# Clustered attention and two mixers: packed one-hot transposes, weighted sums a step later, similarities in one step, denominators per head

## The reference

```python
q_assign = argmax(q_n @ c_n.T)          # per head: 16 clusters, 768 queries, 64 dimensions
k_assign = argmax(k_n @ c_n.T)
mask = q_assign[:, None] == k_assign[None, :]
scores = where(mask, q @ k.T / sqrt(64), -1e9)
attn = softmax(scores)                  # per row
out = attn @ v
```

## Time and profile before

| what | value |
|---|---|
| median of 3 runs | 699.2 us (699.09 to 701.43) |
| the profiled execution | 700.45 us, span of its records 698.6 us |
| TensorE's mean granted clock | 0.993 of full speed |
| busy, share of the span | TensorE 97%, VectorE 56%, ScalarE 48%, GpSimd 27% |
| the attention stage | from some 16 us to 281.5 us |

### The profile page before, as it was taken

How to read it: one execution, slowest core, us unless ns; L and a number is a source line. 1 busy time by engine, 2 the same in 40 slices (tenths; PEclk the granted TensorE clock), 3 DMA queues, 4 the chain that set the end, 5 groups by cost and what they waited for, 6 DMA issues and landing times.

```text
span 698.6 us, 11568 instructions
## 1 busy us (share of the span) xinstructions
PE 679.3 (97%) x4188; PEld 643.6 (92%) x4188; DVE 391.5 (56%) x673; ACT 338.5 (48%) x641; POOL 191.8 (27%) x140
## 2 busy tenths in 40 slices
PE   7999999999999998999999999999999999999998
PEld 6888898989898987889999999999999999999998
DVE  6698888888897988445212202403268626671133
ACT  4687878787978788424401201301277425530010
POOL 5558253443535374402600000200223200060000
PEclk8999999999999999999999999999999999999999
DMA  6474644535353451100300000010231100000022
GB/s 218 87 177 122 170 100 103 135 68 135 68 135 68 100 149 46 32 14 20 125 9 0 1 1 0 0 45 1 59 122 50 57 1 1 0 1 1 1 90 91
DMA packets 16016, 45.44 MB, mean 65 GB/s; under 512 B 2544, under 2 KB 4592, under 8 KB 15984
## 3 DMA queue, kind: packets, MB, share of 16 engines
q1 hardware_dynamic: 15984, 45.00, 23.9%
HBM read 24.15 MB, written 3.15 MB: 39 GB/s over the span
## 4 chain that ended last, share of the span: by engine, by line
PE 87%; ACT 4%; DVE 4%; issue 3%; DMA 0%; ACTq 0%; DVEq 0%; SPq 0%
PE ps L439 19%; PE ps L441 19%; PE ps L440 19%; PE ps L477 7%; PE ps L485 5%; PE ps L469 4%; PE ps L486 4%; PE ps L470 4%; PE ps L450 3%; PE ps L461 1%; DVE pt_lo L1067 1%; ACT pt_hi L758 1%; ACT prob L783 1%; ACT kb L778 1%; PE ps L492 1%
## 5 line engine op out<-in xcount | busy, mean ns | idle before, releaser
L1039 DVE TENSOR_REDUCE neg_max<-ps 128x1 f32<-128x768 f32 x96 | 91.5, 954 | 27.4 <-PE ps L470 24.5
L1067 DVE TENSOR_TENSOR pt_lo<-ps,pt_hi 128x384 fp32r<-128x384 f32 x192 | 97.5, 549 | 11.2 <-ACT pt_hi L758 10.8
L758 ACT ACTIVATE pt_hi<-ps 128x384 fp32r<-128x384 f32 x192 | 84.4, 489 | 38.1 <-PE ps L477 36.6
L783 ACT ACTIVATE prob<-ps,neg_max 128x768 f32<-128x768 f32 x96 | 86.7, 904 | 13.1 <-DVE neg_max L1039 11.9
L867 ACT ACTIVATE g_s<-ps 128x384 fp32r<-128x384 f32 x48 | 23.6, 492 | 139.4 <-PE ps L441 139.4
L441 PE MATMUL ps<-u_s,ch_s 128*128 128x384 f32 (+1 forms) x256 | 85.5, 334 | 0.0
L439 PE MATMUL ps<-u_s,ch_s 128*128 128x384 f32 (+1 forms) x256 | 85.5, 334 | 0.0
L440 PE MATMUL ps<-u_s,ch_s 128*128 128x384 f32 (+1 forms) x256 | 85.5, 334 | 0.0
L477 PE MATMUL ps<-ident,prob 128*128 128x128 f32 x576 | 82.9, 278 | 1.4 <-DVE pt_lo L1067 1.3
L477 PEld LDWEIGHTS ps<-ident,prob 128*128 128x128 f32 x576 | 67.0, 143 | 10.6 <-DVE pt_lo L1067 2.7
L485 PE MATMUL ps<-pt_lo,v_s 128*128 128x384 f32 x192 | 70.2, 366 | 4.8 <-DVE o_sum L1046 4.8
(11 more groups left out here) (143 smaller groups left out, 1419.7 us busy)
## 6 DMA issues: line engine op xcount, KB each, us to landing
stage<-ch_dram SPq DMA_DIRECT2D x9, 768.0 KB, 4.3
qa<-pair_s SPq DMA_DIRECT2D x30, 192.0 KB, 2.8
ka<-pair_s SPq DMA_DIRECT2D x30, 192.0 KB, 3.8
raw<-q_dram SPq DMA_DIRECT2D x8, 384.0 KB, 4.2
raw<-k_dram SPq DMA_DIRECT2D x8, 384.0 KB, 4.6
raw_v<-v_dram SPq DMA_DIRECT2D x8, 384.0 KB, 4.3
out_dram<-act_u SPq DMA_DIRECT2D x16, 192.0 KB, 1.9
qb<-pair_s SPq DMA_DIRECT2D x15, 192.0 KB, 3.4
```

What stands on the lines that cost most here:

```text
L758: return act.activation(o, i, ACT.Copy)
L783: act.activation(prob[:, slot, :].rearrange("p (c k) -> p c k", c=2), ps[:, 2 * slot:2 * slot + 2, 0:HS], ACT.Exp, bias=neg_max[:, s:s + 1 ...
L1039: dve.tensor_reduce(neg_max[:, s:s + 1], ps[:, 2 * slot2:2 * slot2 + 2, 0:HS], AX.XY, ALU.max, negate=True).then_inc(s_max, 1)
L1067: dve.tensor_tensor(pt_lo[at], ps[:, 4 + u, 0:HS].rearrange("p (k q) -> p k q", k=HT), pt_hi[at], ALU.subtract).then_inc(s_pt_lo, 1)
```

## The change

- `onehot` has 32 columns for each of the four combinations of head and side, 16 of them always zero, so that one transpose of 128 columns gives the rows of both heads and both sides. One group of six per pair is left, behind the transposes of step 7.
- ScalarE copies all 128 rows at once to a new tile `oh_rows` (`rows_out`, with scale and bias from small per-partition tiles, function Identity), and SyncE's `oh_in` copies 16 rows each to qb and kb of the two heads: four transfers a pair. Only for the very first head the rows are still copied by ScalarE itself.
- In TensorE's order part 0 of `weighted_v` goes from the end of steps t = 0 and 3 to steps t = 1 and 4, between the scores and the transposes; part 1 goes from the end of t = 1 and 4 to the start of t = 2 and 5, ahead of the scores.
- Both sides of `sims` are in step 3, one ahead of the transposes and one behind. VectorE's argmax steps go from steps 3, 4, 5, 6, 7 to 3, 3, 3, 4, 6.
- rden holds the six tiles of a head, made at t = 0 of the next head by `denominators`; `x_out` waits for that and for s_x_bank.

```diff
-                onehot = sb(a1, "onehot", [P, 2, NT, 2, C], BF16)
+                onehot = sb(a1, "onehot", [P, NT, 2, 2, 2 * C], BF16)
+                oh_rows = sb(a1, "oh_rows", [P, S], F32R)
...
+            def oh_in(p, j):
+                sp.wait_ge(s_oh_rows, p + 1)
+                for dst, side in ((qb, 0), (kb, 1)):
+                    r = j * D + side * 2 * C
+                    sp.dma_start(dst[D:D + C, j, :].bitcast(F32), oh_rows[r:r + C, :].bitcast(F32)
+                                 ).then_inc(s_oh_in[j], 16)
+
...
+                oh_in(p + 1, 0)
                 sp.wait_ge(s_score, 12 * p + 12)
                 stack(p + 1, 1)
+                oh_in(p + 1, 1)
 
...
-                pool.wait_ge(s_rden, n + 1)
+                pool.wait_ge(s_x_bank, n + 1)
+                pool.wait_ge(s_rden, 2 * p + j + 1)
                 pool.tensor_tensor(x_tok[:, bass.ds(p * NT + half * HT, HT), j * D:(j + 1) * D], o_sum[:, half, :, :],
-                                   rden[:, half, :].unsqueeze(2).broadcast_to([P, HT, D]),
+                                   rden[:, j, half * HT:half * HT + HT].unsqueeze(2).broadcast_to([P, HT, D]),
                                    ALU.mult).then_inc(s_x, 1)
 
...
+                    pe.wait_ge(s_oh_rows, p)
                     pe.wait_ge(s_cen_t, 4)
                     pe.wait_ge(s_qk_c, p)
...
-            def oh_transpose(j, side, bank=7):
-
-                rows = ps[D:D + C, bank, 0:HS].bitcast(BF16)
+            def oh_transpose(bank=7):
+
+                rows = ps[:, bank, 0:HS].bitcast(BF16)
                 for t in range(NT):
-                    mm = pe.transpose(rows[:, t * P:(t + 1) * P], onehot[:, side, t, j, :], identb[:])
+                    mm = pe.transpose(rows[:, t * P:(t + 1) * P],
+                                      onehot[:, t, :, :, :].rearrange("p j s c -> p (j s c)"), identb[:])
                 mm.then_inc(s_oh_t, 1)
 
...
+            def second_half_v(n, j, part):
+
+                pe.wait_ge(s_pt_lo, 6 * n - 1 + part)
+                if part == 0:
+                    pe.wait_ge(s_x_bank, n - 1)
+                weighted_v(1 - j, 1, part)
+
+            def first_half_v(p, n, j, part, prev):
+
+                pe.wait_ge(s_pt_lo, 6 * n + 5 + part)
+                if part == 0:
+                    pe.wait_ge(s_v_split, 2 * p + j + 1)
+                    if prev:
+                        pe.wait_ge(s_x_bank, n)
+                weighted_v(j, 0, part)
 
             def pair(p, first=False, last=False):
                 for s in range(12):
                     j, t = s // NT, s % NT
                     g = 12 * p + s
                     n = 4 * p + 2 * j
+                    prev = not (first and j == 0)
+                    if t == 2 and prev:
+                        second_half_v(n, j, 1)
+                    if t == 5:
+                        first_half_v(p, n, j, 1, prev)
                     if not (last and s >= 10):
                         next_score(p, s + 2)
-                    if s == 0:
-                        pe.wait_ge(s_koh, 2 * p + 1)
-                        oh_transpose(1, 0)
                     if s == 3 and not last:
-                        sims(p + 1, 1)
-                    prev = not (first and j == 0)
+                        sims(p + 1, 0)
+                    if t == 1 and prev:
+                        second_half_v(n, j, 0)
+                    if t == 4:
+                        first_half_v(p, n, j, 0, prev)
                     pe.wait_ge(s_exp, g + 1)
                     for u in range(2):
                         if not (first and s == 0):
                             pe.wait_ge(s_pt_lo, 2 * g + u - 1)
                         transposes(g, s % 2, u)
-                    if s == 1:
-                        pe.wait_ge(s_qoh, 2 * p + 2)
-                        oh_transpose(1, 1)
-                    if s == 2 and not last:
-                        pe.wait_ge(s_koh, 2 * p + 2)
-                        sims(p + 1, 0)
-                    if s == 8 and not last:
+                    if s == 3 and not last:
+                        sims(p + 1, 1)
+                    if s == 7 and not last:
                         pe.wait_ge(s_onehot, p + 3)
-                        oh_transpose(0, 0)
-                    if s == 9 and not last:
-                        pe.wait_ge(s_qoh, 2 * p + 3)
-                        oh_transpose(0, 1)
+                        oh_transpose()
                     if (t == 2 and prev) or t == 5:
                         pe.wait_ge(s_ot, n if t == 2 else n + 1)
                         o_transpose()
-
-                    if prev and t < 2:
-                        pe.wait_ge(s_pt_lo, 6 * n - 1 + t)
-                        if t == 0:
-                            pe.wait_ge(s_x_bank, n - 1)
-                        weighted_v(1 - j, 1, t)
-                    if t in (3, 4):
-                        pe.wait_ge(s_pt_lo, 6 * n + 5 + t - 3)
-                        if t == 3:
-                            pe.wait_ge(s_v_split, 2 * p + j + 1)
-                            if prev:
-                                pe.wait_ge(s_x_bank, n)
-                        weighted_v(j, 0, t - 3)
 
             def idle_work(n):
                 for i in range(n):
...
-            def query_rows(h, j, bank=7):
-                act.wait_ge(s_oh_t, 2 * h + 1)
-                copy(qb[D:D + C, j, :], ps[D:D + C, bank, 0:HS].bitcast(BF16)).then_inc(s_qoh, 1)
-
-            def mask_rows(h, j, bank=7):
-
-                act.wait_ge(s_oh_t, 2 * h + 2)
-                act.activation(kb[D:D + C, j, :], ps[D:D + C, bank, 0:HS].bitcast(BF16), ACT.Copy,
+            def query_rows_first():
+                act.wait_ge(s_oh_t, 1)
+                copy(qb[D:D + C, 0, :], ps[0:C, 6, 0:HS].bitcast(BF16)).then_inc(s_qoh, 1)
+
+            def mask_rows_first():
+
+                act.wait_ge(s_oh_t, 2)
+                act.activation(kb[D:D + C, 0, :], ps[2 * C:3 * C, 5, 0:HS].bitcast(BF16), ACT.Copy,
                                scale=BIG, bias=-BIG).then_inc(s_koh, 1)
+
+            def rows_out(p, bank=7):
+
+                act.wait_ge(s_oh_t, p + 2)
+                act.activation(oh_rows[:], ps[:, bank, 0:HS].bitcast(BF16), ACT.Identity, scale=oh_scale[:, 0:1],
+                               bias=oh_bias[:, 0:1]).then_inc(s_oh_rows, 1)
 
...
-                    if s == 0:
-                        query_rows(2 * p + 1, 1)
-                    if s == 1:
-                        mask_rows(2 * p + 1, 1)
-                    if s == 8 and not last:
-                        query_rows(2 * p + 2, 0)
-                    if s == 9 and not last:
-                        mask_rows(2 * p + 2, 0)
-
-            query_rows(0, 0, bank=6)
-            mask_rows(0, 0, bank=5)
+                    if s == 7 and not last:
+                        if not first:
+                            act.wait_ge(s_oh_in[0], 32 * p)
+                        act.wait_ge(s_oh_in[1], 32 * p + 32)
+                        rows_out(p + 1)
+
+            act.wait_ge(s_oh_zero, 9)
+            query_rows_first()
+            mask_rows_first()
+            rows_out(0, bank=5)
...
+            dve.memset(onehot[:], 0.0).then_inc(s_oh_zero, 1)
+            for r in range(4):
+                rows = slice(2 * C * r, 2 * C * r + 2 * C)
+                dve.memset(oh_scale[rows, :], BIG if r % 2 else 1.0).then_inc(s_oh_zero, 1)
+                dve.memset(oh_bias[rows, :], -BIG if r % 2 else 0.0).then_inc(s_oh_zero, 1)
...
-            def half_out(n, half, j):
+            def half_out(n, half):
 
                 dve.wait_ge(s_ott, n + 1)
-                if half is not None:
-                    dve.tensor_reduce(o_sum[:, half, :, :],
-                                      ps[:, 6, 0:HS].rearrange("p (t a d) -> p t d a", t=HT, a=2), AX.X,
-                                      ALU.add).then_inc(s_x_bank, 1)
-                s = NT * j + HT * half
-                dve.tensor_scalar(rden[:, half, :], den[:, s:s + HT], 1e-9, None, ALU.add).then_inc(s_den, 1)
-                dve.wait_ge(s_den, n + 1)
-                dve.reciprocal(rden[:, half, :], rden[:, half, :]).then_inc(s_rden, 1)
+                dve.tensor_reduce(o_sum[:, half, :, :], ps[:, 6, 0:HS].rearrange("p (t a d) -> p t d a", t=HT, a=2),
+                                  AX.X, ALU.add).then_inc(s_x_bank, 1)
+
+            def denominators(h, j):
+                dve.tensor_scalar(rden[:, j, :], den[:, NT * j:NT * j + NT], 1e-9, None, ALU.add).then_inc(s_den, 1)
+                dve.wait_ge(s_den, h + 1)
+                dve.reciprocal(rden[:, j, :], rden[:, j, :]).then_inc(s_rden, 1)
 
             def pair(p, first=False, last=False):
                 for s in range(12):
                     n = 4 * p + 2 * j
                     if not (last and s >= 10):
                         row_max(g + 2, s % 2, (s + 2) % 12)
-                    if s == 7 and not last:
```

(20 more changed lines are left out.)

45 lines of the change are left out of this document (27 added, 18 removed).

## The result

The changed kernel takes 679.12 us (median of 4 runs, 678.63 to 680.13), the kernel before beside it 699.51 (699.09 to 701.43). The ratio is 0.9711, with a 95% interval of 0.970 to 0.972: 20.4 us less. The prediction said 681.5, 17.7 less than the 699.2 that it started from. The profiled executions, 700.45 and 680.13 us, differ by 20.3.

The account below looks back on a forecast made before the run. TensorE, busy 97% of the span, was taken as the bound. Full pairs save 2.4 x 7 = 16.8 us, the last pair 1.2, the start costs 0.3: 17.7 off 699.2 gives 681.5 us, range 676 to 691.

Parts of the forecast that it names:

- main term: Attention stage: a full pair of heads takes 30.3 us against 32.7, saving 2.4 us in each of seven pairs, 16.8.
- Packed one-hot transposes: TensorE, attention pairs: 32 groups of six transposes become nine, 14.3 us off; wider loads give 0.5 us back.
- ScalarE's copies: ScalarE, row copies: one 1.0 us copy replaces four of 0.80 a pair, 2.2 us less; Identity loads no table.
- Rival 4: ScalarE, row copy: Identity needs another table, two 1.28 us loads a pair; 6 us slower, 705; chance 0.04 including the like.
- Copies by DMA: SyncE's row transfers to qb and kb: landing in 1.9 to 2.5 us, no cost but little room for head 0.
- rival 3: Row transfers come late: landing at 4.1 us costs 1.5 us a pair, 10 us, total 692; chance 0.08.
- wrong if S(12) waits for the rows: Sign against the forecast: the next pair's first score products on TensorE wait for transferred key rows; no such wait was forecast.
- V one step later: TensorE's weighted sums: moving part 0 behind the next scores removes the 0.47 us wait for o_sum at step 6.
- All similarities in step 3: TensorE similarities, VectorE argmax lump: TensorE's 2.5 us a pair stay; waits in a pair 1.0 us, today 1.6.
- Denominators per head: VectorE: two pairs of small instructions instead of four save 0.6 us a pair; GpSimd's later x_out is hidden.
- Start and end: Before the first pair: zeroing onehot (0.5 us) and eight memsets cost 0 to 0.5 us; last pair's end keeps its order.

## Why the prediction was right, and where its working was not

**The total** was 2.4 us from the measured one, and its main term was right in mechanism: the period fell to 29.9, where 30.3 was worked out. In the sum, the group with the stretch of the T ahead stood at 0.7 and takes 0.32, its late start being among the waits; the waits are 0.66 for 1.0. That is 0.7 less. The rest was counted as 26.1 + 2.5 and is 0.3 more: the T between the two sides of the similarities takes 0.68 (120.73 to 121.41) and the S behind them 0.80, and T and O of step 8 take 0.71 and 0.30, where 0.58, 0.71, 0.65 and 0.25 were the prices.

**Step "Packed one-hot transposes"**, 14.3 us off TensorE. The work did go. But that this step pays by itself was wrong with the addition in place: alone it gives 2.3 us, and 12 to 13 without the addition on either side. The working took TensorE's own sum and one estimate of the waits for the whole, and did not ask whether VectorE would still be in time if only TensorE became shorter. The price of the group was bounded by 0.43 and 0.58 and lies below both: the wide load costs less than the narrow one.

**Step "ScalarE's copies".** 1.0 was the estimate, 0.99 the measurement. Identity loads no table. The whole trace has three loads, at 0.74, 16.88 and 490.26 us, as the kernel before has (0.74, 16.12, 511.91). Only the second lies in the attention stage, and the eight Identity copies, one at 15.88 and seven among the exponentials, add none. Rival 4 falls with it.

```profile
16.88 1.28 ACT L811 ACT_TABLE_LOAD   x1
```

The rule of the Trainium skill, page ScalarE: Activation LUTs, section on table sets, was weighed in the prediction; the trace now agrees with it for Identity as well as for copy.

**Step "Copies by DMA"**, "no cost, but little room". Right but for one pair (landing 2.1 us, room 0.3). In the second pair rival 3 happened: landing 5.6 us, a wait of 3.03. By the prediction's own signs ("wrong if S(12) waits for the rows") this pair speaks against it. The working counted the queue from a steady pair; the second pair still has GpSimd's weight splits ahead of split_qk. Its pair takes 33.19, with the weight early 29.87, and so gained 0.5 instead of 2.4.

**Step "V one step later"**, "takes away the 0.47". The place of V is worth 0.47, but that is luck. In the kernel before the move does take away the wait for o_sum; in the changed kernel the order of o_sum and argmax has already done so, and what the move saves is wait of T for pt_lo, which the step said would get no more room. Not foreseen either: the same edit costs 10 us in the kernel before, since V covered the wait for the key rows. In the changed kernel one group at step 7 replaces the two at steps 8 and 9, and the rows are there 0.3 ahead of S(12) without that cover.

**Step "All similarities in step 3"**. T(6), the one-hot group, T(0) and T(9) wait 0.16, 0.26, 0.17 and 0.07, where 0.15, 0.4, 0.2 and 0.2 were counted. The lump was taken as a neutral exchange, and spreading it costs 0.8 a pair: its place is part of the gain.

**Step "Denominators per head"** is the one that failed in size: 0.6 us of VectorE a pair, hidden, nothing on the path. Undoing it costs 12.4 us, 10.9 of them through the addition's lock with GpSimd and what follows from it; without the addition the place of the denominators is worth nothing in a steady pair (29.8 either way). The step read the mean of the reciprocal and put the sum ahead of it at "somewhat less", when the addition's longest was 1672 ns against a median of 159.

**Step "Start and end"**, -0.3. The zeroing takes 0.38 us and is hidden; up to step 11 of the first pair 3.35 are won, not 2.1, and the last pair gives 2.1, not 1.2. Part of the first is the addition's and the clock's: the kernel before has one addition of 1.67 us ahead of that place and the 3.4 us at the lower clock, and without both it reaches it at 51.17 instead of 51.96. The other 0.5 was not traced. In the last pair a wait of 0.45 for pt_lo is gone too, and the kernel before gains 0.3 there without the addition; the rest was not traced.

**Why the total came out near.** Partly by luck: the second pair fell short by 1.9, and the other pairs and the first stretch gave more than was counted. Where the gain of a steady pair comes from is seen best without the addition, in four kernels that differ by one step each: the kernel before 32.58, with the packing (and argmax behind o_sum) 30.93, with V and the lump as well 29.80, with the denominators per head 29.9. So the packing gives 1.65 and V and the lump together 1.1. Undone one at a time in the changed kernel, V and the lump cost 0.47 and 0.8; these overlap by a little. The last of the four still has its addition, which is locked once in the whole run (0.47 us at 52 us).

## What to carry to other kernels

Work taken off the bounding engine pays only as far as the next engine keeps up: sum each neighbour's chain for every part of an edit alone, and ask of each piece of work that is moved what it was covering. Look at the longest of a tiny instruction beside its median; where they differ tenfold, something holds it, and what holds it may come more often when the rest gets faster. A stop of the bounding engine can cost more than its length, by the clock behind it. And a number that agrees is no proof of its cause: look whether the wait that was to go has come back when the edit is undone. Count a queue in the first pairs too, where the start's work still lies ahead of it.

## What the runs showed of the hardware that was not expected

- A tensor_scalar of VectorE over 128 x 3 elements in SBUF takes 0.16 us, and 3.45 when GpSimd's 3.46 us instruction on SBUF began just before; it ends with it. The reciprocal of the same tile was never longer than 0.19. The Trainium skill, page SBUF — State Buffer, section Who interferes with whom, says that a tensor_scalar can run in a mode that needs the port pair shared with GpSimd, and that whoever comes second is blocked for the whole instruction; the trace agrees (3.45 beside 3.46).
- Six bf16 transposes cost less with 128 columns loaded and 128 rows written than with 16: 0.33 against 0.43, and the T ahead 0.66 against 0.75. Why the narrow load pauses is not settled.
- ScalarE's Identity with scale and bias read per partition takes 0.99 us over 128 x 768 elements; its Copy with constants for both takes 0.80 over 16 x 768.
- A 48 KB transfer within SBUF lands 2.1 us after its issue with nothing else under way, and 5.6 behind the stack, v, q and k.
- TensorE's granted clock fell to 0.50 at or just behind six stops: for 3.4 us at stops of 2.06, 2.08 and 3.25 us for pt_lo and of 3.05 us for the rows, for 6.8 us at stops of 3.00 us for pt_lo and 4.78 us for the rows. In the changed kernel it stayed at 1.00 behind a stop of 3.03 us. What decides is not shown.
